# Gate logits from the gated activations instead of from the rows of x2, and the expert routing placed inside the second dense layer's products

## What is computed

```
attention   state = gamma * state + k v^T ;  y = scale * q state        (8 heads of 64)
dense       h  = relu(x @ w_in)                                         (512 -> 1024)
            c  = 3-tap convolution of h along the tokens, one filter per column
            x2 = (h * sigmoid(c)) @ w_out                               (1024 -> 512)
experts     logits = x2 @ w_gate (8 columns), local = sigmoid(x2 @ w_local)
            e(s) = argmax(logits) at s = 0 or where local < 0.5, else e(s-1)
            out  = softmax(logits)[e] * (relu(x2 @ w1[e]) @ w2[e])
```

## Time and profile before

| what | us |
|---|---|
| median of 3 runs | 462.82 (459.57 to 462.93) |
| the profiled execution: its own time | 460.67 |
| the profiled execution: span in the trace | 458.8 |
| first layer of batch 0 starts | 59.79 |
| second layer of batch 0 starts | 93.18 |
| batch 1 starts | 136.01 |
| last matmul of the logits ends, routing begins | about 212.3 |
| first product of expert 0 | 237.86 |

### The profile page before, as it was taken

The page is one execution under the profiler, slowest core; times in us unless marked ns, Lnnn a source line. Parts: engine busy times, 40 slices in busy tenths (PEclk is TensorE's granted clock), DMA queues, the critical chain, the costliest instruction groups (busy, mean ns, idle before and its releaser), DMA issues.

```text
span 458.8 us, 7520 instructions
## 1 busy us (share of the span) xinstructions
PE 432.2 (94%) x2673; PEld 363.5 (79%) x2674; DVE 218.4 (48%) x284; ACT 200.9 (44%) x275; POOL 187.8 (41%) x145
## 2 busy tenths in 40 slices
PE   5999799999999999997778999999999999999993
PEld 2888699988879998885446888888888888888872
DVE  2489629990214995124841542221672263535440
ACT  2235478752115873442032552222882273645550
POOL 3422964433000444590241282211676246363761
PEclk9599999999999999999599999999999999999998
DMA  8999200001010000926346119111177605638110
GB/s 313 430 364 326 127 1 2 0 1 69 23 47 0 0 0 7 366 106 242 149 154 281 48 34 401 43 46 47 46 279 280 270 23 187 250 127 324 31 28 13
DMA packets 12583, 62.94 MB, mean 137 GB/s; under 512 B 2256, under 2 KB 2512, under 8 KB 8209
## 3 DMA queue, kind: packets, MB, share of 16 engines
q1 hardware_dynamic: 9648, 54.51, 30.4%
q0 software_dynamic: 2912, 8.13, 5.5%
HBM read 56.34 MB, written 7.60 MB: 139 GB/s over the span
## 4 chain that ended last, share of the span: by engine, by line
PE 85%; DMA 4%; POOL 4%; DVE 2%; issue 2%; ACT 1%; SPq 1%; POOLq 0%; DVEq 0%
PE ps L887 23%; PE ps L889 22%; PE ps L888 22%; PE ps L1091 3%; PE ps L880 2%; DMA kv<-qkv 2%; PE ps L977 2%; DMA xg<-x_rows,gnow 2%; POOL win L362 2%; PE ps L934 2%; PE ps L913 2%; PE ps L931 2%; PE ps L1057 2%; PE ps L971 1%; PE ps L899 1%
## 5 line engine op out<-in xcount | busy, mean ns | idle before, releaser
L394 POOL TENSOR_TENSOR wx<-raw_w,wx 128x1024 fp32r<-128x1024 f32 x29 | 72.5, 2519 | 20.9 <-ACT wx L525 20.7
L525 ACT CAST wx<-raw_w 128x1024 fp32r<-128x1024 f32 x64 | 62.7, 1057 | 17.5 <-DVE sidx L803 14.6
L385 POOL TENSOR_TENSOR hg<-cv,hg 128x768 fp32r<-128x768 f32 x16 | 31.3, 1960 | 79.3 <-ACT hg L547 79.3
L887 PE MATMUL ps<-wx,xT 128*128 128x512 f32 x136 | 54.4, 400 | 2.5 <-DVE xT L822 2.5
L887 PE MATMUL ps<-wx,hT 128*128 128x512 f32 x136 | 54.5, 401 | 0.7 <-POOL wx L394 0.7
L889 PE MATMUL ps<-wx,hT 128*128 128x512 f32 x136 | 53.2, 391 | 0.0
L889 PE MATMUL ps<-wx,xT 128*128 128x512 f32 x136 | 53.1, 391 | 0.0
L888 PE MATMUL ps<-wx,hT 128*128 128x512 f32 x136 | 53.1, 390 | 0.0
L888 PE MATMUL ps<-wx,xT 128*128 128x512 f32 x136 | 53.0, 390 | 0.0
L822 DVE TENSOR_TENSOR xT<-ps,xT 128x512 fp32r<-128x512 f32 x18 | 12.4, 692 | 67.8 <-ACT xT L569 67.8
L813 DVE TENSOR_TENSOR wx<-raw_w,wx 128x1024 fp32r<-128x1024 f32 x35 | 41.2, 1227 | 5.4 <-ACT wx L525 5.1
(11 more groups left out here) (141 smaller groups left out, 817.1 us busy)
## 6 DMA issues: line engine op xcount, KB each, us to landing
raw_w<-w_exp SPq DMA_DIRECT2D x32, 1024.0 KB, 7.6
qk<-qkv SPq DMA_DIRECT2D x8, 768.0 KB, 6.9
kv<-qkv SPq DMA_DIRECT2D x8, 768.0 KB, 8.4
x_rows<-x2n SPq DMA_DIRECT2D x12, 256.0 KB, 2.1
win_raw<-w_in SPq DMA_DIRECT2D x1, 2048.0 KB, 21.6
wout_raw<-w_out SPq DMA_DIRECT2D x1, 2048.0 KB, 10.5
decay<-decay_c SPq DMA_DIRECT2D x1, 576.0 KB, 7.4
xg<-x_rows,gnow POOLq DMA_INDIRECT x19
```

Of the source, the lines that this page charges most:

```text
L385: nc.gpsimd.tensor_tensor(hg[:, 1, f, :], cv[f % 4][:], hg[:, 0, f, :].bitcast(F32), ALU.subtract).then_inc(hglo_done, 1)
L394: ins = nc.gpsimd.tensor_tensor(wx[:, slot, 1, c], raw, wx[:, slot, 0, c].bitcast(F32), ALU.subtract)
L525: nc.scalar.copy(wx[:, slot, 0, c], raw).then_inc(wx_hi[w], 1)
L887: mm(o, lh, rl, start=first, stop=False)
```

## The change

Four things are done together.

1. **Logits.** Instead of x2 times gate weights, the kernel forms `w2g = w_out @ w_gl` once, on chip, and multiplies the gated activations by it. `w_out` is loaded a second time, transposed (`woutT`, 2 MB, ahead of `wout_raw` in SP's queue). `gate_first` makes 8 fp32 matmuls of 512 columns before the first dense product, each with 32 output rows, four of them side by side in the partitions of psW; ACT copies the result (`wgp`); `gate_second`, after the first block of the first layer, adds the four strips with 8 matmuls of 9 columns, and DVE makes hi and lo of it (`w2g`, in columns 0 to 8 and 64 to 72 of 80). Then `logits(b, f)` is 4 matmuls of 384 columns with w2g as the stationary operand; in each batch five such groups stand between first-layer blocks (after block f comes `logits(b, f - 3)`), three between second-layer products. One DVE copy, 6 small matmuls (`turn_logits`) and one more copy give a batch's logits. The transposes, their copies and the 6 groups of small products per batch go.
2. **The subtraction for hg lo** moves from POOL to DVE, which now has four instructions for each block.
3. **Second layer.** The six token blocks have psX banks 4, 5, 0, 1, 4, 5.
4. **Routing** of both batches is placed inside batch 1's second layer. ACT rounds expert 0's w1 ahead of it and its w2 within; POOL does six of expert 0's eight subtractions ahead of the payloads and two behind. Expert 0's raw weights get places of their own (`raw_first`, loaded once the first layer is done). The loops over the batches are unrolled; warm-ups stand only at the end (24), before the experts.

```diff
@@ PE
+            def gate_first():
+                pe.wait_ge(small_in, 32)
+                pe.wait_ge(wt_in, 16)
+                for a in range(2):
+                    for k in range(KD):
+                        last = mm(psW[WG * k:WG * k + WG, 512 * a:512 * a + 512], wgl[:, k, :],
+                                  woutT[:, k, 512 * a:512 * a + 512], start=True, stop=True)
+                last.then_inc(wg_mm, 1)
+            def gate_second():
+                pe.wait_ge(wgp_done, 1)
...
+                    last = mm(psG[:, (E + 1) * f:(E + 1) * f + E + 1], wgp[:, P * f:P * f + P],
+                              con[:, C_SELW:C_SELW + E + 1], start=True, stop=True)
+            def logits(b, f):
+                pe.wait_ge(hglo_done, KF * b + f + 1)
+                for a in range(2):
+                    for w in range(2):
+                        last = mm(psL[:, a, :], w2g[:, f, :], hg[:, w, f, HALF * a:HALF * a + HALF],
+                                  start=(f == 0 and w == 0), stop=(f == KF - 1 and w == 1))
...
+            for b in range(B):
+                if b == 0:
+                    pe.wait_ge(ylo_done, 2 * B * NP_)
+                    gate_first()
+                for f in range(KF):
...
+                    last.then_inc(hp_done, 1)
+                    if u == 0:
+                        gate_second()
+                        pe.wait_ge(w2g_done, 2)
+                    if b and f == 3:
+                        pe.wait_ge(lg_done, b)
+                    if f >= 3:
+                        logits(b, f - 3)
...
+                for k in range(KF):
+                    pe.wait_ge(hglo_done, KF * b + k + 1)
...
+                    if k in (1, 3, 4):
+                        logits(b, {1: KF - 3, 3: KF - 2, 4: KF - 1}[k])
+                    if k == 5:
+                        turn_logits(b)
+                    if b == B - 1 and k == 6:
+                        keep_rows()
+                if b == B - 1:
+                    code_rows()
+                for j in range(3, TB):
+                    if j >= 4:
+                        pe.wait_ge(x2_out, TB * b + j - 3)
+                    for k in range(KF):
+                        x2_part(j, k)
+                        if b == B - 1:
+                            if (j, k) == (3, 6):
+                                totals()
+                            if (j, k) == (3, 7):
+                                offsets()
+                            if (j, k) == (4, 1):
+                                slots()
+                            if (j, k) == (5, 0):
+                                inverse()
+            warm_up(24, bank(7))
@@ ACT
+            act.wait_ge(wg_mm, 1)
+            nc.scalar.copy(wgp[:], psW).then_inc(wgp_done, 1)
...
+                if b == B - 1:
+                    act.wait_ge(hp_done, B * KF)
+                    weights_hi(0, 0, 0)
+                    act.wait_ge(r_keeps, 1)
...
+                    if b == B - 1 and j == 2:
+                        weights_hi(1, 0, 0)
@@ DVE
+                    if f >= 2:
+                        dve.wait_ge(hghi_done, KF * b + f - 1)
+                        nc.vector.tensor_tensor(hg[:, 1, f - 2, :], cv[(f - 2) % 4][:], hg[:, 0, f - 2, :].bitcast(F32),
+                                                ALU.subtract).then_inc(hglo_done, 1)
@@ POOL
-            weights_lo(1, 0, 0, range(4))
+            weights_lo(1, 0, 0, (0, 1))
...
+            weights_lo(1, 0, 0, (2, 3))
```

More of the change, by code:

```diff
@@ L65 @@
 C_GC = C_KDEC + H
-C_END = C_GC + NP_ * (CH - 1)
+C_SELW = C_GC + NP_ * (CH - 1)
+C_SELL = C_SELW + E + 1
+C_END = C_SELL + E + 1
+WG = 32
+LR = 80
+LO_ROW = 64
 def constants():
@@ L127, in build @@
     wout_raw = at("wout_raw", [P, KF * DM], F32, 96)
+    woutT = at("woutT", [P, KD, FF], F32, 80)
+    wgp = at("wgp", [P, FF], F32, 112)
+    lgr = at("lgr", [LR, S], F32, 186)
     hg = at("hg", [P, 2, KF, S], F32R, 112)
@@ L624, in _ @@
             nc.vector.memset(warm[:], 0.0).then_inc(made, 1)
+            nc.vector.memset(w2g[:].bitcast(F32), 0.0).then_inc(made, 1)
             nc.vector.memset(cmb[:], 0.0).then_inc(made, 1)
@@ L1012, in _ @@
-            pe.wait_ge(made, 5)
-            for ps_rows, cols, ready, done in ((psKeep, kpb, r_keep_in, r_keeps), (psCode, cmb, r_code_in, r_codes)):
+            def gate_first():
[6 more added lines that the diff above has]
+                last.then_inc(wg_mm, 1)
@@ new lines, in turn_logits, with x2_part @@
+            def turn_logits(b):
+                pe.wait_ge(lr_done, b + 1)
+                for j in range(TB):
+                    last = mm(psLT[:, (E + 1) * j:(E + 1) * j + E + 1], lgr[:, P * j:P * j + P],
+                              con[0:LR, C_SELL:C_SELL + E + 1], start=True, stop=True)
+                last.then_inc(lg_mm, 1)
+            def x2_part(j, k):
+                ts = slice(P * j, P * j + P)
+                ws = slice(DM * k, DM * k + DM)
+                last = three(psX[j], hg[:, 0, k, ts], hg[:, 1, k, ts], wout[:, 0, ws], wout[:, 1, ws],
+                             k == 0, k == KF - 1)
+                if k == KF - 1:
+                    last.then_inc(x2_done, 1)
@@ L1014, in _, with to_rows @@
+            def to_rows(ps_rows, cols, ready, done):
                 pe.wait_ge(ready, 1)
@@ L1042, in _, with keep_rows @@
-            warm_up(12, bank(5))
-            pe.wait_ge(r_pay, 1)
-            for i in range(TT):
-                if i % 3 == 0:
-                    pe.wait_ge(r_rhot, i // 3 + 1)
-                last = mm(psInv[:, 0:3 * NG], rhot[:, i, :], pay[:, i].rearrange("p a g -> p (a g)"),
-                          start=(i == 0), stop=(i == TT - 1))
-            last.then_inc(r_inv, 1)
-            warm_up(18, bank(5))
+            def keep_rows():
+                pe.wait_ge(made, 6)
+                pe.wait_ge(relu_done, B * KF)
+                to_rows(psKeep, kpb, r_keep_in, r_keeps)
@@ new lines, in slots @@
+            def slots():
+                pe.wait_ge(r_slotrow, 1)
+                for i in range(TB):
+                    last = mm(psSlot[:, BE * i:BE * i + BE], slot_r[:, P * i:P * i + P], idr[:], start=True, stop=True)
+                last.then_inc(r_slots, 1)
+                pe.wait_ge(r_tab_in, 1)
+                mm(psRow[0:1, 8:8 + E], small[0:E, 2:3], con[0:E, C_ID:C_ID + E], start=True, stop=True)
+                mm(psRow[0:1, 8 + E:9 + E], small[0:E, 1:2], con[0:E, C_ID + E - 1:C_ID + E], start=True,
+                   stop=True).then_inc(r_tabs, 1)
```

270 lines of the change are left out of this document (126 added, 144 removed).

## The result

| | before | after |
|---|---|---|
| median, us (runs) | 462.88 (4) | 475.20 (4, 474.47 to 476.82) |
| ratio | | 1.0297, 95% interval 1.0265 to 1.0330 |
| span of the profiled execution | 458.8 | 474.9 |

The changed kernel is 3% slower: 12.3 us by the two medians, 13.7 by the ratio on 462 us, where 2.3 were forecast against the median (4.5 on the profiled execution). The profiled execution of after is the slowest of its four, 16.1 us over before by the spans.

The account below looks back on a forecast made before the run. TensorE, busy 432 of 458.8 us, was taken as the bound. Start +7.4, arithmetic -6.9, hg lo +8.4, routing -7.9 and clock +3.5 sum to +4.5 on 460.67: 465.2 us, range 457 to 470.

Parts of the forecast that it names:

- The start: First layer of batch 0: waiting for all of x1, gate_first 3.8, gate_second and its wait for DVE 2.3; +7.4 us.
- strip after strip: In gate_first: matmuls issued one strip after another, taken as 3.8 us; four strips side by side would give 1.8.
- Arithmetic: Both batches' two layers with logits: 72.8 us each where 76.2 before; -6.9 us in all.
- the wait for hg lo: Logits groups wait for DVE's subtraction, ready 5.9 us after a block: 1.7 once, 1.0 twice per batch; +8.4 us.
- Routing: Routing inside batch 1's second layer and the tail behind it: 25.6 us becomes 17.7, so -7.9.
- I charge 1.6 in all; ends 0.3 and 6: TensorE's waits for DVE's routing chain inside batch 1's second layer: 1.6 us, between 0.3 and 6.
- the third rival: In the routing, POOL's subtractions block DVE; two further instructions hit: +4 us, 469.2. Chance 0.2.
- the 0.6 of cover: In the second layer, the running count is ready at 25.5 us, TensorE gets to totals at 26.1: 0.6 spare.
- The order of POOL's work: Six of expert 0's eight POOL subtractions lie around the routing; each blocked DVE instruction costs up to 2.5 us.
- The tail: From the second layer's end through store, gather and transposes to expert 0's first product: 10.0 plus 0.7, so 10.7 us.
- The clock: Ahead of expert 0: half speed for 10.2 us after an idle time, slowing some 7 us of products; +3.5, ends 0 and 5.
- the prediction's own marks: Times foretold: second block at 71.4, second layers about 108 and 185, last x2 product near 228, expert 0 near 239.

Follow-up runs that it names:

- e1: Changed kernel with POOL's four subtractions for expert 0's w2 moved out of the routing, two behind the gather table, two behind the first gather: 462.83 us, ratio 1.0036.
- e6: Changed kernel with only the two POOL subtractions beside comparison and running count moved behind the gather table: 469.84 us, ratio 1.0179.
- e2: Changed kernel with each logits group one block later, block f followed by the group of block f - 4: 468.12 us, ratio 1.0144.
- e7: Changed kernel with only the two POOL subtractions behind the payloads, beside the one-hot rows, taken away: 468.58 us, ratio 1.0136.
- e10: e5 plus 40 warm-ups, w2g wait ahead of first logits, expert 2's w1 load after first gather, xT lo before expert 1's w1: 455.05 us.
- e4: Changed kernel with 40 warm-ups instead of 24 ahead of the experts: 473.59 us, ratio 1.0246.
- e5: Changed kernel with the edits of e1 and e2 together: 456.74 us, ratio 0.9904.
- e8: Changed kernel with e2's logits, routing and old warm-ups behind the second layer again, POOL's eight subtractions ahead of the payloads: 461.53 us, ratio 0.9990.
- e11: e5 with the subtraction for hg lo back on POOL: 456.87 us, ratio 0.9900.
- e3: Changed kernel with gate_first behind block 0, the second gate product behind block 1, w2g wait ahead of the first logits: 478.56 us, ratio 1.0369.

## Why the prediction was wrong, point by point

- **The start (forecast +7.4).** Block 1 of the first layer starts at 70.49; by the prediction, 71.4. `gate_first` took 1.9 us, not 3.8, and the wait for w2g was 0.7 as forecast. But attention ended 0.8 later, at half clock, and block 1 itself ran at half clock for 3.4 us, 1.7 lost. Both were missing terms; together they made up for the first, by luck: neither stretch is in the profiled executions of e1 and e6, whose code up to there is the same.

```profile
61.82 1.92 PE L978 MATMUL ps<-woutT,wgl 128*32 128x512 f32 x16 [1.16 <-DVE x L677]
67.95 1.85 PE L986 MATMUL ps<-con,wgp 128*128 128x9 f32 x16
70.49 0.69 PE L907 MATMUL ps<-x,win 128*128 128x384 f32 x1 [0.69 <-DVE w2g L701]
```

  The Trainium skill's factor of 4 (TensorEngine Tiling (Array Packing), Theoretical Speedup) is what the trace shows: 16 instructions in 1.92, against the estimate of 1.8 that a factor of 4 gives from the earlier trace rows. My reading, strip after strip, was the wrong one.
- **Arithmetic and the wait for hg lo (-6.9 and +8.4).** Right. Six waits, 6.6 us in all, each 1.65 or 0.85 as derived (1.7 and 1.0); e2 took them away and gained 7.1. The sum had a slip: with 0.1 for a restart the waits of 1.0 are 1.1 each and not 1.2, so the term was 8.0. Batch 1 starts at 145.08 (144.2 forecast), its second layer at 185.94 (185.3).
- **Routing (-7.9).** This step failed. "I charge 1.6 in all; ends 0.3 and 6" was the sum's term for waits inside the second layer. They were 7.2 us, 5.6 more, and some 10 us of the layer ran at half clock, which is 5.1 lost; the two together are the 10.8 by which the layer missed (53.8 for 43). The mechanism was the third rival's, with a chance of 0.2 and a price of +4: too cheap, for two reasons. I counted the waiting and not the clock behind it (e6 and e7: the layer is 5.6 and 6.1 us shorter for 3.5 and 3.7 of waiting). And I left the comparison (L769) out of the list of blocked instructions, while it lost 2.2 us. With the 2.0 of the running count that is 4.2, less the 0.6 of cover 3.6; TensorE waited 3.5. The Trainium skill (SBUF — State Buffer, Who interferes with whom) has the comparison too: beside DVE instructions with two SBUF inputs it names `tensor_scalar` in a two-port mode among those that share a port with POOL. The trace agrees: 2.77 for 0.61, and 0.61 again in e1.
- **The order of POOL's work.** The prediction did have POOL's pieces at the right places, but treated each as one possible hit. The trace has two pairs and both hit fully: in each, one DVE instruction got through per POOL instruction, so the four one-hot instructions went from 2.77 to 7.08.
- **The tail (10.7).** 12.35. The gather took 4.6, where 4.0 were allowed for; the index copy took 1.19 for 0.18, beside DVE's subtractions for expert 1. In e10, with those moved behind it, it took 0.18.
- **The clock (+3.5).** Its place was right (0.50 from 248 to 255), its price too high: from the first product to the second block's it cost 1.3 (10.0 for 8.7), as only 2.9 us of the stretch lay over products.

The span's 16.1 us, by the prediction's own marks: 4.5 forecast; second layer +10.8; tail +1.7; start and batches +0.6; expert stage's first block 2.2 less; 0.6 further on. The rest, about 0.1, is rounding.

## What to carry to other kernels

Before a second engine's chain is laid inside TensorE's work, look at what POOL does at that time: DVE instructions with two inputs in SBUF, and the comparison here, waited for POOL's whole subtraction, and a chain of short DVE steps then moves at POOL's pace. When work is interleaved, give each consumer the full latency of its producer in TensorE blocks (here four blocks and not three). Price a wait of TensorE with the slow clock that may follow: here waits of 3.5 and 3.7 us cost 1.6 to 1.7 times their length, and the short ones for hg lo about their length.

## What the runs showed of the hardware that I had not expected

- DVE and POOL block each other in both directions: POOL's index copy took 1.19 us beside DVE's weight subtraction and 0.18 without (e10). A DVE copy that reads PSUM took 0.95 beside POOL and 0.95 without.
- The same code does not always meet the same clock. Behind 16 instructions of 9 columns and a wait of 0.7 us the clock fell to 0.50 for 3.4 us in the profiled executions of the changed kernel, e2, e4, e5, e8 and e11, and stayed at 1.00 in those of e1, e6 and e7. The end of attention fell into a stretch of 3.4 us in the changed kernel, e3 and e7 and in none of the other nine, whose code up to there is the same. What decides that stays open. Other slow stretches here last up to 10.2 us.
- Four fp32 matmuls with 32 output rows each run side by side, although each is two instructions: 16 instructions of 512 columns took 1.92 us, 0.96 for each group of four. For a pair with 64 rows give an estimate of 0.88.
